# One declaration moved in on-chip memory: the weight-piece buffer `pairs` goes below the FFN's staging and input buffers

## The reference

```
state+= : y[t] = r[t] @ (state + (u*k[t]) v[t]^T);  state = w*state + k[t] v[t]^T
logits  = x @ w_gate + modality_bias[modality_id];  e = argmax(logits)
x       = softmax(logits)[e] * (relu(x @ w1[e]) @ w2[e])
xn      = x / sqrt(mean(x*x) + 1e-6) * rms_g
out     = (silu(xn @ w_gate2) * (xn @ w_val)) @ w_out        # 384 -> 1536 -> 384
```

## The kernel before

| tensor | bytes per partition | start before | remainder by 64 | start after the change | remainder by 64 |
|---|---|---|---|---|---|
| pairs | 30720 | 75680 | 32 | 56192 | 0 |
| ffn_raw, o_sb0 | 4608, 1536 | 56192 | 0 | 86912 | 0 |
| o_sb1 | 1536 | 57728 | 0 | 88448 | 0 |
| w_sum | 2560 | 60800 | 0 | 91520 | 0 |
| staged | 10240 | 63360 | 0 | 94080 | 0 |
| y_in | 12320 | 63360 | 0 | 94080 | 0 |

## Time and profile before

### The profile page before, as it was taken

One profiled execution on the slowest core, in us unless ns is written; L12 is line 12 of the kernel. 1 busy time (PEld: TensorE's weight loads), 2 busy tenths in 40 slices (PEclk: granted clock), 3 DMA queues, 4 the chain that ended last, 5 costly groups with the idle time before them and its releaser, 6 DMA issues.

```text
span 816.5 us, 14845 instructions
## 1 busy us (share of the span) xinstructions
PE 793.2 (97%) x5145; PEld 723.0 (89%) x5145; DVE 495.8 (61%) x917; ACT 360.0 (44%) x859; POOL 147.6 (18%) x144
## 2 busy tenths in 40 slices
PE   8999997998999999999999999999999999999998
PEld 6898885798999999998789988988998898899888
DVE  6899998853435534424876287567528756732871
ACT  6787786553546544533442242234224223422420
POOL 5897671221122222211000000000000000000000
PEclk9999999999999999999999999999999999999999
DMA  8898851526447633440642145434214513421301
GB/s 254 257 267 256 250 182 52 201 88 246 174 160 282 218 132 132 135 165 25 206 160 99 50 152 196 136 138 162 98 54 150 193 59 139 165 94 55 139 10 68
DMA packets 35233, 122.42 MB, mean 150 GB/s; under 512 B 5202, under 2 KB 17774, under 8 KB 29408
## 3 DMA queue, kind: packets, MB, share of 16 engines
q1 hardware_dynamic: 30656, 111.70, 39.6%
q0 software_dynamic: 3328, 9.45, 3.9%
q10 hardware_dynamic: 1184, 0.45, 0.2%
HBM read 92.09 MB, written 30.29 MB: 150 GB/s over the span
## 4 chain that ended last, share of the span: by engine, by line
PE 84%; DVE 6%; issue 3%; DMA 3%; ACT 2%; POOL 1%; DVEq 0%; SPq 0%; ACTq 0%; POOLq 0%
PE bank L1708 42%; PE bank L1773 33%; PE bank L1589 2%; DVE rkt L1045 2%; PE bank L1599 2%; PE bank L1625 1%; DMA ffn_s<-pairs 1%; DMA rkn_in<-rk_n 1%; PE bank L1643 1%; PE bank L1764 1%; PE bank L1701 1%; PE bank L1638 1%; ACT am L800 1%; DVE bonus L1052 0%; POOL ru L671 0%
## 5 line engine op out<-in xcount | busy, mean ns | idle before, releaser
L1773 PE MATMUL bank<-x_hi,pairs 128*128 128x512 f32 x792 | 244.8, 390 | 1.2 <-DVE second L1450 0.8
L1773 PEld LDWEIGHTS bank<-x_hi,pairs 128*128 128x128 f32 x792 | 148.0, 188 | 34.2 <-DVE second L1450 1.7
L1773 PE MATMUL bank<-x_lo,pairs 128*128 128x512 f32 x396 | 154.1, 389 | 0.0
L1708 PE MATMUL bank<-out_hi,hh 128*128 128x384 f32 x288 | 97.3, 338 | 0.0
L1708 PE MATMUL bank<-out_hi,hl 128*128 128x384 f32 x288 | 96.8, 336 | 0.0
L1708 PE MATMUL bank<-out_lo,hh 128*128 128x384 f32 x288 | 96.8, 336 | 0.0
L1349 DVE SCALAR_TENSOR_TENSOR h_lo<-bank,h_hi 128x512 fp32r<-128x512 f32 (+1 forms) x52 | 34.6, 670 | 101.2 <-ACT h_hi L880 101.2
L1708 PE MATMUL bank<-xg_hi,w_hi 128*128 128x256 f32 (+1 forms) x312 | 88.3, 283 | 0.9 <-DVEq L1336 0.8
L1708 PE MATMUL bank<-xg_hi,w_lo 128*128 128x256 f32 (+1 forms) x312 | 88.1, 282 | 0.0
L1708 PE MATMUL bank<-xg_lo,w_hi 128*128 128x256 f32 (+1 forms) x312 | 88.1, 282 | 0.0
L1773 PEld LDWEIGHTS bank<-x_lo,pairs 128*128 128x128 f32 x396 | 74.3, 188 | 15.5
(11 more groups left out here) (240 smaller groups left out, 1390.5 us busy)
## 6 DMA issues: line engine op xcount, KB each, us to landing
pairs<-ffn_s SPq DMA_DIRECT2D x33, 1280.0 KB, 5.5
ffn_s<-staged SPq DMA_DIRECT2D x9, 1280.0 KB, 4.9
rk_in<-rk_t SPq DMA_DIRECT2D x24, 448.0 KB, 4.4
rkn_in<-rk_n SPq DMA_DIRECT2D x24, 384.0 KB, 4.7
ffn_raw<-ffn_w SPq DMA_DIRECT2D x12, 576.0 KB, 5.4
w_raw<-w SPq DMA_DIRECT2D x16, 384.0 KB, 4.4
y_in<-y_tok SPq DMA_DIRECT2D x3, 1540.0 KB, 7.1
v_in<-v_n SPq DMA_DIRECT2D x24, 192.0 KB, 4.1
```

The costliest lines, as they stand in the source:

```text
L1708: last = pe.matmul(dst, left[a], right[b2], start=first and n == 0, stop=end and n == 2)
L1773: last = pe.matmul(dst, pair[:, w, a, :], (x_hi, x_lo)[h][:, x, :], start=first and n == 0, stop=n == 2, skip_group_check=True)
```

## The change

The declaration of `pairs` moves from behind `y_in` to ahead of the stack `pieces_end`, so `pairs` lies directly behind `out_lo`, and `ffn_raw`, `w_sum`, `staged`, `o_sb0`, `o_sb1` and `y_in` lie 30720 bytes higher. No instruction, semaphore, loop or DMA is added, taken away or put elsewhere: the order of instructions on PE, DVE, ACT, POOL and SP is the same row for row, and only operand addresses differ.

```diff
         out_hi = sb("out_hi", [P, FFC, DM], F32R)
         out_lo = sb("out_lo", [P, FFC, DM], F32R)
+        pairs = sb("pairs", [P, SLOTS, 2, FG], F32R)
         pieces_end = ExitStack()
         ffn_raw = sb("ffn_raw", [P, FW], F32, pieces_end)
         w_sum = sb("w_sum", [P, WT - WD, P], F32, pieces_end)
...
         o_sb = [sb(f"o_sb{i}", [P, DM]) for i in range(2)]
         sb("rest_of_raw", [P, FW + (WT - WD) * P - 2 * DM])
         y_in = sb("y_in", [P, FS, YW])
-        pairs = sb("pairs", [P, SLOTS, 2, FG], F32R)
         first_1 = [sb(f"first_1{i}", [P, FB]) for i in range(2)]
```

## The result

The changed kernel takes 825.26 us in the median of 20 runs, against 818.89 us for the kernel before: ratio 1.0079, 95% interval 1.0050 to 1.0107. (One of the 20 runs of before took 4453 us; without it the median is 818.82, and that gives the ratio.) It is slower by 0.8%. That is within the 1% that I called "same", but it is clear of 1.000, and it lies outside the range of 813.2 to 823.3.

The account below looks back on a forecast made before the run. The prediction took PE to bound the kernel and put the terms for PE's weight reads, ACT and DVE writes, other movers and DMAs at 0 each, leaving 818.3 us, with a range of 813.2 to 823.3.

Parts of the forecast that it names:

- What bounds the kernel: Whole kernel: PE, busy 793.2 of 816.5 us; an edit shows only through matmul cost or PE's few waits.
- PE reading `pairs` as weights: FFN's 1188 matmuls with weights from pairs: no added cost, 0 us, at most 0.6 us either way.
- Three places: Matmuls on pairs, output products and down: 13.3, 13.3 and 13.8 ns beside the columns, so remainders by 64 add 0.
- The weight loads of 188 ns: PE's loads from pairs, hh and h_hi: median 188 ns each at remainders 32, 32 and 0, offered as confirming equal cost.
- ACT and DVE: Their writes of pieces into pairs and staged take the same at both; term 0, possible difference 0.05 us.
- DMAs: Loads of pairs have 9.0 us of cover; the uncovered store pair stays at 10.02 us; term 0, bounds -5.1 to +5.0.
- The rule on transactions that start at multiples of 256 bytes: Stores from pairs: rows of 325 beats become 324, shrinking the 10.02 us landing by 0.03 us.
- (a): Stores of pieces 0 and 1 land earlier and ACT never waits: -5.1 us, 813.2 us; chance 0.03.
- (d): Stores of pieces 0 and 1 land later by up to 5.0 us: 823.3 us; chance 0.05.
- (b): PE's weights from a start at a multiple of 64 cost less: at best 15.8 us, 802.5 us; chance 0.03.
- (c): FFN matmuls slowed by pairs' new neighbourhood: +15.8 us, 834.1 us, visible as slower from 6.9 ns each; chance 0.06.
- The Trainium skill's rule on cachelines: Operand reads from pairs: both starts are multiples of 16 bytes, so equal lines are crossed, sum 0.

Follow-up runs that it names:

- grid_7: Changed kernel with x_hi, x_lo at 160 by 256, slots at -8, -24 and 0 bytes, hh, hl moved to out_hi's remainder: 233.3, 231.1, 226.8 ns; ratio 1.0059.
- b_ffn32: Kernel before with 32 bytes of filler ahead of x_hi, pairs unmoved: matmuls reading pairs 233.3 ns, 144 output products 25.44 us instead of 24.96.
- grid_5: Changed kernel with x_hi and x_lo both at 128 by 256, slots of pairs at 128, 160, 96: 227.0, 233.3, 233.4 ns.
- a_off32: Changed kernel with 32 bytes of filler ahead of pairs, which then starts at 56224: 226.7 ns a matmul, ratio to before 1.0031.
- grid_4: Changed kernel with x_hi, x_lo unmoved and slots 4, 16 and -16 bytes off the cheap place: 232.3, 231.5, 227.2 ns.
- grid_1: Changed kernel with slots at 0, 32, 96 by 128, x_hi at 0, x_lo at 64, hh at 0, hl at 32: 231.9, 233.3, 235.5 ns.
- grid_3: Changed kernel with x_hi, x_lo unmoved and slots at distances 128, 256 and 64 by 512 from them: 232.5, 226.7, 233.2 ns.

## Why the prediction was wrong

**What bounds the kernel.** Right: the whole difference is the cost of PE's matmuls, and PE remains busy for 97% of the span.

**PE reading `pairs` as weights: the step that failed.** I put this term at 1188 x 0, with 0.6 us as the most that the rows left. It measured 6.6 ns a matmul: 7.8 us if all 1188 pay it, 6.55 us seen over 990 of them, 6.4 us in the medians. The step that failed is "Three places, both remainders for weights and both for moving operands, and the cost of each is the same to half a nanosecond". I had looked at each operand's remainder by itself, and the rows did cover those. But the cost goes by the two starts together. By distance the three places were 0 for `pairs` and `x_hi`, +32 for `hh` and `out_hi` and +32 for `h_hi` and `w2_hi`, and the two at +32 had 384 columns, not 512. At 384 columns +32 costs nothing (and 0 neither, `grid_7`), while +64 costs 2.5 ns (173.4 to 175.9 from start to start in the mean, `b_ffn32`). So no row of before had 512 columns at any distance but 0, the very thing that the change made. The last paragraph of the prediction named this gap ("where two operands lie relative to each other") and gave it no share of its own. That the total still fell within 1% is luck: the 6.6 ns happened to be just under the 6.9 that would have made it "slower", and nothing in the forecast foresaw them.

The kernel before is, by this measure, at the best distance. The change moved `pairs` 19488 bytes down; by 256 that is a distance of -32.

**The weight loads of 188 ns** were no evidence. They are 187 and 188 ns in the cheap and in the dear kernels. The duration of a load, and the modelled end of a matmul, say little about the pace; the starts do.

**ACT and DVE.** Right: their totals are 360.2 and 496.5 us, before 360.0 and 495.8. (The 229280 in that paragraph is the end of `part_o`, which ACT and DVE use; PE's operands end at 224192, with `h_lo`.)

**DMAs.** Right. The two stores landed after 9.91 us (before 10.02), and ACT waited 4.44 us for them:

```profile
193.91 0.74 ACT L902 ACTIVATE staged<-ffn_raw 128x640 fp32r<-128x640 f32 x1 [4.44 <-DMA ffn_s<-pairs]
```

The slowest load of `pairs` landed after 7.1 us, later than the 6 of the forecast, but 7.9 of the 15.0 us until the slot is wanted were left:

```profile
DMA to landing us min/median/max: 5.1/5.4/7.1
```

The rule on transactions that start at multiples of 256 bytes (the Trainium skill, "DMA: Bandwidth & Descriptors", "How a descriptor splits into AXI transactions") would by the estimate of the prediction have taken 0.03 us off; no run here can show that.

**The rivals.** (a) and (d), the stores landing earlier or later: no. (b), weights at multiples of 64 cost less: no; such a start cost 233.3 ns in the changed kernel and 227.0 in `grid_5`, where the moving operand starts at the same remainder. (c), a collision: right in kind, the time of a matmul by where its operands lie, and its point of decision of 6.9 ns was all but reached with 6.6. It was wrong in its picture (regions and neighbours, `a_off32`) and I had taken the price from a surplus that is not this one: the 13.3 ns are there in the best case too. Its chance of 0.06 was too small, since all that spoke against it, beside the old place itself, were rows at another column count.

**The Trainium skill's rule on cachelines** of 16 bytes ("SBUF — State Buffer", "Specifications (TRN2)") gave a sum of 0, and the measurement differs: both starts are multiples of 16 and the cost is not the same. The same page, section "Who interferes with whom", calls the ports of PE for the moving operand and for the weights independent. They may be, but the pace of matmuls here changes by 3% with the distance of the two starts, and with neither start alone.

What stays open is the mechanism. Two reads of one core that meet in the same part of the memory, with a pattern of 256 bytes, would give such a table; that is argued, not shown. The table has no simple form (-64 is cheaper than +64, -16 than -8), I did not separate the columns from it (384 columns have another table than 512), and at +16 and -16 the same two starts give more than one pace.

## What to carry to other kernels

Where PE is the bound, the start of the stationary operand against that of the moving operand is a tuning parameter: here 32 bytes are worth 3% of a matmul of 512 columns, and 6.4 us of 818 in the medians. Moving a tensor in a list of declarations changes it without a word in the code, so compare starts by 256 bytes before and after, and put a filler in where they differ. And a row from the trace is evidence for another place only if it has the same shape and the same relation of both operands; read a matmul's cost from the distance of starts, not from durations.

## What the runs showed of the hardware

- The cost of a matmul of 512 columns in 4-byte values, in a row of such with a weight load each, is 226.7 ns at best and 233.3 at worst in this table, at the full granted clock. Its mean over a group goes with the distance of weights and moving operand by 256 bytes, and at 0, -64, +32 and -32 the same distance in other places repeats to 0.3 ns. At +16 single groups have 226.7 or 233.3 ns with the same two starts (`grid_4`).
- It is not a cost per access that adds up evenly. In `grid_1`, where the two moving operands had different remainders, the means reached 235.5 ns, more than any single distance gives; and `pair_a` there, at 0 from `x_hi` and -64 from `x_lo`, cost 231.9 ns, where the table's 226.7 and 229.0 would give 227.5.
- At 384 columns distances 0 and +32 cost the same, 173.5 and 173.4 ns, and +64 costs 175.9.
- A wait of PE of 0.8 to 0.9 us in the last expert tile is followed in some executions by half the granted clock for some 14 us (changed, `grid_1`, `grid_3`, `grid_4`), and in others not at all (before, `b_ffn32`, `grid_7`). It costs 18.93 - 12.48 = 6.5 us, as much as the change itself.
